# Softmax of the first three batches: one exponential instruction for a round, or one for each head straight from the scores

## What is computed

```python
# q, k, v: (8 batches, 8 heads, 576 positions, 64 columns)
k_p = k.reshape(B, H, 72, 8, D).mean(axis=3)
v_p = v.reshape(B, H, 72, 8, D).mean(axis=3)
scores = scale * np.matmul(q, k_p.transpose(0, 1, 3, 2))      # scale = 1 / sqrt(64)
scores = scores - np.max(scores, axis=-1, keepdims=True)
attn = np.exp(scores)
attn = attn / (np.sum(attn, axis=-1, keepdims=True) + 1e-09)
out = np.matmul(attn, v_p)                                     # 576 x 64 for each head
# x = out as (4608 tokens, 512); y = ((x @ w1) * (x @ w2)) @ w3 @ w_out
# then: expert = argmax of the gate, y2 = gate * (relu(y @ w1[e]) @ w2[e])
```

## Time and profile before

| | us |
|---|---|
| median of 3 runs | 1170.06 |
| lowest and highest run | 1167.63, 1171.43 |
| the profiled execution | 1171.54 |
| its span, first to last instruction | 1169.7 |
| TensorE busy in the span | 1140.0 |
| VectorE busy | 676.1 |
| ScalarE busy | 398.5 |
| GpSimd busy | 557.5 |

### The profile page before, as it was taken

One profiled execution on the slowest core, in us unless ns is written; L12 is line 12 of the kernel. 1 busy time (PEld: TensorE's weight loads), 2 busy tenths in 40 slices (PEclk: granted clock), 3 DMA queues, 4 the chain that ended last, 5 costly groups with the idle time before them and its releaser, 6 DMA issues.

```text
span 1169.7 us, 29725 instructions
## 1 busy us (share of the span) xinstructions
PE 1140.0 (97%) x11982; PEld 1069.5 (91%) x11983; DVE 676.1 (58%) x1260; ACT 398.5 (34%) x906; POOL 557.5 (48%) x565
## 2 busy tenths in 40 slices
PE   8899989999999999999999999999999999999997
PEld 7688889999999999999999999999899899999986
DVE  0799798898988874662544456733433445433332
ACT  1566455655555552333322224211111132111111
POOL 2254866677767645550000002167645545645544
PEclk9999999999999999999999999999999999999999
DMA  9765363636536334344444447234111111111111
GB/s 348 272 180 141 113 183 97 192 103 181 167 92 205 88 80 111 113 127 131 131 133 136 136 136 243 63 105 154 49 45 54 45 36 42 49 45 51 48 45 46
DMA packets 103779, 137.88 MB, mean 118 GB/s; under 512 B 20083, under 2 KB 70003, under 8 KB 103668
## 3 DMA queue, kind: packets, MB, share of 16 engines
q1 hardware_dynamic: 41060, 79.51, 21.6%
q10 hardware_dynamic: 53040, 36.29, 10.7%
q0 software_dynamic: 9568, 20.51, 5.7%
HBM read 93.58 MB, written 43.21 MB: 117 GB/s over the span
## 4 chain that ended last, share of the span: by engine, by line
PE 53%; DMA 1%; POOL 0%; issue 0%; DVE 0%; ACT 0%; ACTq 0%; POOLq 0%; DVEq 0%
PE ab L777 6%; PE ab L776 6%; PE ab L778 6%; PE x2p L776 6%; PE rt L777 6%; PE rt L776 6%; PE rt L778 6%; PE x2p L778 6%; PE x2p L777 6%; DMA g_rows<-gst 1%; DMA xg<-x_rows,idx_c 0%; PE ab L956 0%; POOL gst L659 0%; DMA out<-y_out,tok_c 0%; PE sct L966 0%
## 5 line engine op out<-in xcount | busy, mean ns | idle before, releaser
L745 POOL DMA_INDIRECT xq<-x_rows,idx_q x152 | 145.2, 955 | 55.6 <-issue 39.9
L777 PE MATMUL ab<-xtl,e1h 128*128 128x256 f32 x608 | 170.5, 281 | 0.0
L776 PE MATMUL ab<-xth,e1h 128*128 128x256 f32 x608 | 169.5, 279 | 0.0
L778 PE MATMUL ab<-xth,e1l 128*128 128x256 f32 x608 | 169.2, 278 | 0.0
L2069 DVE SCALAR_TENSOR_TENSOR htl<-ab,hth 128x512 fp32r<-128x512 f32 x76 | 52.4, 691 | 155.9 <-ACT hth L1453 155.8
L1453 ACT ACTIVATE hth<-ab 128x512 fp32r<-128x512 f32 x76 | 45.4, 598 | 276.4 <-PE ab L778 276.4
L776 PEld LDWEIGHTS ab<-xth,e1h 128*128 128x128 f32 x608 | 114.1, 188 | 1.0 <-issue 0.4
L777 PEld LDWEIGHTS ab<-xtl,e1h 128*128 128x128 f32 x608 | 114.4, 188 | 0.7
L778 PEld LDWEIGHTS ab<-xth,e1l 128*128 128x128 f32 x608 | 114.2, 188 | 0.0
L1132 ACT ACTIVATE pb<-pb,rc 128x72 f32<-128x72 f32 x320 | 83.2, 348 | 60.0 <-DVE rc L1527 60.0
L776 PE MATMUL x2p<-xh,wh 128*128 128x256 f32 x336 | 97.5, 290 | 2.9 <-DVE kb L1566 2.5
(11 more groups left out here) (236 smaller groups left out, 3475.8 us busy)
## 6 DMA issues: line engine op xcount, KB each, us to landing
gr<-g_rows SPq DMA_DIRECT2D x36, 512.0 KB, 3.7
kv<-in_v SPq DMA_DIRECT2D x24, 512.0 KB, 4.2
qt<-in_q ACTq DMA_DIRECT2D x38, 256.0 KB, 3.4
kv<-in_k SPq DMA_DIRECT2D x16, 576.0 KB, 5.2
g_rows<-gst ACTq DMA_DIRECT2D x72, 128.0 KB, 2.7
g_rows<-gst ACTq DMA_DIRECT2D x36, 256.0 KB, 3.2
x_rows<-xr SPq DMA_DIRECT2D x36, 256.0 KB, 2.2
stage<-in_moe_w SPq DMA_DIRECT2D x8, 1024.0 KB, 7.2
```

Source lines behind the costliest of these rows:

```text
L745: pool.indirect_dma_start(out=xq[:, r, g, :], out_offset=None, in_=x_quarters, in_offset=bass.IndirectOffsetOnAxis(ap=idx_q[:, r, n, half: ...
L776: pe.matmul(outp, lh, rh, start=first, stop=False)
L777: pe.matmul(outp, lh, rl, start=False, stop=False)
L778: return pe.matmul(outp, ll, rh, start=False, stop=last)
```

## The change

Rounds with `r < 15`, those of batches 0, 1 and 2, take another way through steps 2 to 4. VectorE takes the maximum and then multiplies it by minus the scale (128x8). It no longer subtracts. ScalarE computes the exponentials in eight instructions, one for each head, with `sct` in PSUM as input, the negative maximum as bias, and the sum over the head's 72 keys as a second result into `sm`. VectorE no longer sums. `sct` is free again only when the eighth exponential has finished, so `may_score` waits for `exp_done` in these rounds. The wait for `p_turned`, which keeps `pb` from being overwritten, moves from VectorE's `soft_max` to ScalarE's `exp_p`. From round 15 on everything is as before; the semaphore has a new name.

```diff
+EARLY = 3 * AT
+SCALE = D ** -0.5 / POOL
...
         # may_score, on TensorE
-                if r:
-                    pe.wait_ge(sub_done, r)
+                if 0 < r <= EARLY:
+                    pe.wait_ge(exp_done, r)
+                if r > EARLY:
+                    pe.wait_ge(max_taken, r)
...
         # weigh_v, on TensorE
-                        pe.wait_ge(sub_done, AT * (b + 1) + 1)
+                        pe.wait_ge(max_taken, AT * (b + 1) + 1)
...
         # exp_p, on ScalarE
-                act.wait_ge(sub_done, r + 1)
-                act.activation(pb[r % 2][:, :], pb[r % 2][:, :], ACT.Exp, scale=D ** -0.5 / POOL).then_inc(exp_done, 1)
+                if r < EARLY:
+
+                    act.wait_ge(max_taken, r + 1)
+                    if r > 1:
+                        act.wait_ge(p_turned, r - 1)
+                    for h in range(H):
+                        keys = slice(KEYS * (h % PAIRS), KEYS * (h % PAIRS + 1))
+                        ins = act.activation(pb[r % 2][:, KEYS * h:KEYS * (h + 1)], sct[:, h // PAIRS, keys], ACT.Exp,
+                                             bias=mx[:, h:h + 1], scale=SCALE, accum_out=sm[:, h:h + 1])
+                else:
+                    act.wait_ge(max_taken, r + 1)
+                    ins = act.activation(pb[r % 2][:, :], pb[r % 2][:, :], ACT.Exp, scale=SCALE)
+                ins.then_inc(exp_done, 1)
                 if r + 2 < AT * B:
                     act.dma_start(qt[:, r % 2, :, :], q[r + 2]).then_inc(q_in[r % 2], 16)
...
         # soft_max, on VectorE
-                if r > 1:
+                if r >= EARLY:
                     dve.wait_ge(p_turned, r - 1)
...
                 dve.tensor_reduce(mx3, sc4, AX, ALU.max).then_inc(dve_done, 1)
                 dve.wait_ge(dve_done, own.next())
+                if r < EARLY:
+                    dve.tensor_scalar(mx[:, :], mx[:, :], -SCALE, None, ALU.mult).then_inc(max_taken, 1)
+                    return
                 dve.tensor_tensor(pb[r % 2][:, :].rearrange("p (a n k) -> p a n k", a=2, k=KEYS), sc4,
                                   mx3.unsqueeze(3).to_broadcast([P, 2, PAIRS, KEYS]),
-                                  ALU.subtract).then_inc(sub_done, 1)
+                                  ALU.subtract).then_inc(max_taken, 1)
...
         # soft_sum, on VectorE
-                dve.tensor_reduce(sm[:, :], pb[r % 2][:, :].rearrange("p (h k) -> p h k", k=KEYS), AX,
-                                  ALU.add).then_inc(dve_done, 1)
-                dve.wait_ge(dve_done, own.next())
+                if r >= EARLY:
+                    dve.tensor_reduce(sm[:, :], pb[r % 2][:, :].rearrange("p (h k) -> p h k", k=KEYS), AX,
+                                      ALU.add).then_inc(dve_done, 1)
+                    dve.wait_ge(dve_done, own.next())
```

More of the change, by code:

```diff
@@ L294, in build @@
         scored = sem("scored")
-        sub_done = sem("sub_done")
+        max_taken = sem("max_taken")
         exp_done = sem("exp_done")
```

## The result

The changed kernel takes 1176.33 us in the median of 7 runs (1175.01 to 1180.82), the kernel before 1170.41 in 7. The ratio is 1.0056 with an interval of 1.0041 to 1.0072, which is 6.6 us, 4.8 to 8.4. The direction was forecast, and the time lies in the range, but the forecast was 16 us slower: the size was wrong by more than a factor of two. The profiled execution took 1176.06, its span 1174.3; that is 4.6 us more than the span before, less than the medians say, as single executions differ.

A forecast was written before the change was run, and what follows sets the result against it. TensorE's work was taken to set the end, with sct's release deciding its waits. Batch terms 6.4 + 5.6 + 3.4 = 15.4 us on a span of 1169.7 gave 1185.1, forecast as 1186 us with time around the span; range 1174 to 1199.

The forecast's parts named there:

- E: Time of a round's eight ScalarE exponentials with their sums, taken as 3.2 us, 0.39 each.
- signs of being wrong: A head taking under 0.3 or over 0.5 us, or round (1,1)'s idle time bringing no fall of the clock.
- (a): Round (0,1), batch 0: the score block starts at 50.0 instead of 46.63, +3.4 us.
- (b): Rounds (0,2) to (0,4): the first two keep up, ScalarE falls behind, TensorE waits at (0,4), +1.7 us.
- (c): Transposition of round (0,4), awaited by weigh_v(0,0): late by 6.4 us, of which +1.3 new; nothing comes back.
- (d): Round (1,1), batch 1: hold +3.2, clock fall 1.3 more, short waits give 0.6 back: +3.9 us.
- (e): Rest of batch 1: (1,2), (1,3) just fit; (1,4) +1.1, late copy for the fifth product +0.6 us.
- (f): Batch 2: waits at rounds (2,1), (2,2) and (2,3), partly given back later, in all +3.4 us.
- The second result is free: Rival for the whole kernel: eight exponentials take 2.1 us; +5.5 us, 1175.5; chance 0.20.
- It does not overlap: Rival for the whole kernel: sums do not overlap, eight take 4.3 us; +26 us, 1196; chance 0.25.
- Faster: Rival: VectorE bounds 133 to 175 us and its relief starts TensorE earlier; 1167 us; chance 0.03.
- No change: Rival: existing waits would have stood there anyway and overtake most of the lag; +2, 1172 us; chance 0.07.

The follow-up runs named there:

- e7: Changed kernel without the second result (accum_out left out), VectorE summing in all rounds: ratio 1.0045, +5.3 us against the kernel before.
- e5: Changed kernel with an unused 128x1 ScalarE copy behind each of the eight exponentials: ratio 1.0109, +12.8 us against the kernel before.
- e2: Kernel before with the change in the five rounds of batch 1 alone: ratio 1.0025, +2.9 us.
- e1: Kernel before with the change in the five rounds of batch 0 alone: ratio 1.0021, +2.5 us.
- e11: Kernel before with two GpSimd value sums moved later, queries' load before the exponential, and e6's edit in batches 1 and 2: ratio 1.0079, +9.2 us.
- e6: Kernel before, subtraction kept and freeing sct; rounds 0 to 14 take eight in-place exponentials with sums from pb, no VectorE sum: ratio 1.0007, +0.8 us.
- e12b: Kernel e6 with TensorE waiting in rounds 1 to 15 for the eighth exponential: ratio 1.0041, +5.3 us against the kernel before.
- e10: Kernel before with the load of round r + 2's queries issued ahead of the exponential in all 40 rounds: ratio 1.0055, +6.4 us.
- e4: Kernel before with TensorE waiting in rounds 1 to 15 for the one exponential instead of the subtraction: ratio 1.0015, +1.8 us.

## Why the prediction was right in direction and wrong in size

**The wrong step is the size of E.** "I take 0.13 more, 0.39 each, E = 3.2 us" was both times too much. The base was 0.21, not 0.26 (e7). L1132 is a copy in SBUF with its scale from a tile; its eight starts are 0.25 apart, those of the exponentials from PSUM 0.21. Which of the differences makes it is not shown. The second result was 0.09, not 0.13 (the changed kernel at 0.30 against e7 at 0.21). E is 2.37 us. Between the prediction's own two ends, 5.5 us at E = 2.1 and 15.4 at 3.2, the walk would have given 8 at this E, which agrees with the measured 4.8 to 8.4. That agreement is partly luck: by batches it would be 3.8, 2.9 and 1.2, and the lags were 3.9, -1.2 and 3.1, so that an error of 4 us in batch 1 and one of 2 us the other way in batch 2 partly cancel. Run e5 brought E near what the prediction had assumed and lost 12.8 instead of 15.4. Both of the prediction's signs of being wrong had come: a head took just under 0.3 us, and the idle time of (1,1) brought no fall of the clock.

**(a)** The mechanism held: score (0,1) waits for the eighth head. +2.0 where 3.4 was said. E's 0.8, a negation 0.3 shorter, and VectorE that came to the maximum 0.5 us sooner are 1.6, a little more than the difference. **(b)** +1.7 at (0,4) did not come; with E = 2.37 the eighth head ended at 67.36 and TensorE came at 67.60. It came at +1.9 in e5. **(c)** The chain to the transposition of (0,4) was late by 3.9 instead of 6.4. Its own part, 1.5 behind score (0,4), was forecast as 1.3.

**(d) and (e)**, batch 1, were wrong for a second reason. The prediction carried batch 0's lag along in full and let the hold add to it, with a fall of the clock. In its own frame (d) was near: with batch 1 alone (e2) the idle time at (1,1) was 3.19 us, the clock fell, and 3.7 us were lost up to score (1,2), where (d) had 3.9, if with the larger E. What failed is the sum with batch 0. "VectorE's `lo_w` and `lo_x` follow it in order and set TensorE's pace until 89, so nothing comes back" was false. Those five `lo_w` took 8.56 us in the kernel before, 7.87 in e1, 6.59 in the changed kernel, 5.99 in e5 and 5.71 in e11, while GpSimd was busy 8.25, 6.64, 3.08, 1.45 and 0 us beside them. GpSimd's sums start when their loads land (the pair at 76.92 in the changed kernel had waited 1.19 us for its load), so a late VectorE meets less of them. From the end of the transposition to the maximum of (1,0) VectorE took 16.5 us before, 15.6 in e1 and 14.5 in the changed kernel, and in e1 the lag shrank by that 0.95 us at (1,1). Batch 0's lag also takes the place of part of the hold (e2 against the changed kernel): in the changed kernel the idle time at (1,1) was 1.80 us and brought no fall of the clock, 1.00 granted from 85 to 133 us. In e5 it was 2.54 us, again with 1.00 behind it. The 1.1 and 0.6 us of (e) did not come in the changed kernel. How the 3.6 us by which the walk is too high in e5 divide between these is not shown.
The Trainium skill (SBUF — State Buffer, Who interferes with whom) says that a VectorE instruction with two SBUF inputs contends with a GpSimd instruction that reads SBUF, and this is the form of `lo_w`. The trace agrees: 1.14 us each alone (e11), 1.71 beside GpSimd (before). The prediction used that section for the negation only.

**(f)** +3.1 where 3.4 was said. Score (2,2) came 1.9 us and (2,3) 2.5 us later than score (2,0) asks, less than forecast. The clock fell behind the first as in the kernel before. This row by windows of the changed kernel, in the columns explained at run e2, is the stretch of 155 to 158 us:

```profile
155.00:158.00 3.00, 1.74 (x66) 1.57 (x67) 1.12 (x4) 2.53 (x14) 0.00 (x0) 0.54 0.90 175
```

The granted clock is 0.54, near the 1.2 GHz level; in the kernel before it was 0.58 from 152 to 155 us.

**The rivals.** "The second result is free" was nearest in time, for another reason: it has a price, but the base was lower. "It does not overlap" is out by the rows. "Faster" is out: VectorE works 18.8 us less and waits 19.8 us more for exponentials. "No change" was right that a part of a lag is overtaken, wrong about how much.

**The side terms.** The negation lasted 0.17 us in the median and 1.75 at most; I had taken 0.67 mostly, with 1.18 as the limit. "The queries of round r + 2 are issued behind the eighth exponential, 2.5 us later" was wrong too; it was 0.7 after the start of the first. In the changed kernel no score block waits for its queries.

## What to carry to other kernels

When work moves from one engine to another, ask first who frees the shared buffer, and when. Here the same eight instructions on ScalarE cost 0.8 us with the buffer freed early (e6) and 5.3 with it held to the eighth (e12b). A lag is not a constant that is carried along: the engine that comes late can meet less contention, and it uses up the next wait. Price a split into many small instructions by the distance between starts, from rows of the same form (function, source memory, where scale and bias come from), and not by their length.

## What the runs showed of the hardware

The accumulator's reading is a ScalarE row of 0.19 to 0.25 us that delays the next instruction by 0.09 only. Heads of 128x72 start every 0.21 us from PSUM with a bias from a tile and no second result (e7), every 0.30 with the second result (changed kernel), and every 0.25 in place in SBUF with a fixed scale and the second result (e12b).

ScalarE's queue issued a DMA while five exponentials ahead of it had not begun (46.70 against 48.05 for the eighth), although it stands behind the eighth in the program. Where the issue stands ahead of the exponential in the program, the exponential began behind it: issue at 209.68, exponential at 210.10 (e10).

TensorE's granted clock did not follow the length of the idle time ahead of it alone. At score (1,1) it stayed at 1.00 after 1.80 us of idle in the changed kernel, 2.54 in e5 and 2.87 in e12b, and it fell after 1.98 in e4 (0.54 from 96 to 99 us) and 3.19 in e2 (0.59 from 95 to 98 us). In e2 2.13 us of idle ahead of score (0,1) brought no fall (1.00 from 43 to 49 us), and by score (0,2) this execution had gained 1.5 us on the kernel before; in e4 it was 0.67 over the same stretch, with 5.60 us of idle.
